# Attention and two feed-forward blocks on one core: another order of the work, a later copy of the pooled part, and shifted tiles for the last product

## What is computed

```python
out_d = sm_attn(mean4(q), mean4(k), mean4(v))        # attention on 144 pooled positions
attn  = repeat(out_d, 4) + sm_attn(q, k, v, |i - j| < 4)   # plus a local band
u     = x + real(fft(fft(x, axis=1), axis=2))         # x: attn as (4, 576, 512)
y     = u + relu(layernorm(u) @ w_ch1) @ w_ch2        # 512 -> 2048 -> 512
h     = relu(y @ w_in)                                # 512 -> 1024
out   = (h * sigmoid(conv3(h, conv_w))) @ w_out       # 1024 -> 512
```

## Time and profile before

| | us |
|---|---|
| median of 3 runs | 821.42 |
| the three runs | 818.27, 821.73, 821.42 |
| the profiled execution | 818.24 |
| its span, first to last instruction | 816.4 |
| PE busy | 804.5 |
| DVE busy | 447.4 |
| ACT busy | 299.3 |
| POOL busy | 269.8 |

### The profile page before, as it was taken

One profiled execution on the slowest core, in us unless ns is written; L12 is line 12 of the kernel. 1 busy time (PEld: TensorE's weight loads), 2 busy tenths in 40 slices (PEclk: granted clock), 3 DMA queues, 4 the chain that ended last, 5 costly groups with the idle time before them and its releaser, 6 DMA issues.

```text
span 816.4 us, 15990 instructions
## 1 busy us (share of the span) xinstructions
PE 804.5 (99%) x6414; PEld 730.0 (89%) x6414; DVE 447.4 (55%) x862; ACT 299.3 (37%) x879; POOL 269.8 (33%) x363
## 2 busy tenths in 40 slices
...
GB/s 187 230 138 136 45 107 56 70 62 86 61 16 107 38 102 4 155 26 1 28 54 214 62 1 64 1 65 0 65 1 1 1 53 1 64 2 1 53 1 65
DMA packets 79666, 49.52 MB, mean 61 GB/s; under 512 B 60240, under 2 KB 69480, under 8 KB 79592
## 3 DMA queue, kind: packets, MB, share of 16 engines
...
## 4 chain that ended last, share of the span: by engine, by line
PE 96%; DVE 2%; ACT 1%; issue 0%; POOL 0%; DVEq 0%; ACTq 0%
PE banks L834 14%; PE banks L851 14%; PE banks L969 12%; PE banks L986 12%; PE banks L928 11%; PE banks L943 11%; PE banks L792 4%; PE banks L734 3%; PE banks L662 2%; PE banks L648 2%; PE banks L695 2%; PE banks L761 1%; PE banks L681 1%; PE banks L719 1%; PE banks L707 1%; PE banks L821 1%
## 5 line engine op out<-in xcount | busy, mean ns | idle before, releaser
L1524 DVE SCALAR_TENSOR_TENSOR hw<-banks,hw 128x512 fp32r<-128x512 f32 x32 | 22.1, 692 | 122.1 <-ACT hw L1151 122.1
L834 PE MATMUL banks<-unH,w1aH 128*128 128x256 f32 x288 | 86.1, 299 | 0.6 <-DVE hL L1385 0.6
L851 PE MATMUL banks<-hH,w2aH 128*128 128x256 f32 x288 | 86.7, 301 | 0.0
L834 PE MATMUL banks<-unL,w1aH 128*128 128x256 f32 x288 | 81.3, 282 | 0.0
L834 PE MATMUL banks<-unH,w1aL 128*128 128x256 f32 x288 | 81.3, 282 | 0.0
L851 PE MATMUL banks<-hL,w2aH 128*128 128x256 f32 x288 | 81.3, 282 | 0.0
L851 PE MATMUL banks<-hH,w2aL 128*128 128x256 f32 x288 | 81.3, 282 | 0.0
L928 PE MATMUL banks<-unw,w1bH 128*128 128x512 f32 x256 | 78.9, 389 | 0.0
L943 PE MATMUL banks<-hw,w2bH 128*128 128x512 f32 x256 | 78.8, 389 | 0.0
L1754 POOL TENSOR_TENSOR accw<-accw,rstd_bc 128x512 f32<-128x512 f32 (+1 forms) x20 | 23.6, 1205 | 166.0 <-DVE remL L1581 85.2
L1385 DVE SCALAR_TENSOR_TENSOR hL<-banks,hH 128x256 fp32r<-128x256 f32 x80 | 33.7, 422 | 79.8 <-ACT hH L1082 79.7
...
## 6 DMA issues: line engine op xcount, KB each, us to landing
...
```

Source lines behind the costliest of these rows:

```text
L834: last = nc.tensor.matmul(bank[0][:, 0:CT], w[wp][:, t, P * m:P * m + P], (unH, unL)[xp][:, t, :], start=(t == 0 and i == 0), stop=(t == P ...
L851: last = nc.tensor.matmul(bank[1 + d // 2][:, CT * (d % 2):CT * (d % 2) + CT], w[wp][:, m, P * d:P * d + P], (hH, hL)[xp][:, m % 2, :], st ...
```

## The change

Four edits:

- PLAN is another order of the same stages. It has 39 filler matmuls where there were 44; all other stages are there once, as before. The first lines of both orders and the stretch around fold.3 are shown.
- For pairs 4 to 15 weigh.n.0 no longer waits for up_kept, and keep_up waits for weigh.n.0's end (pv_ready) in turn. X is then read by ACT only after both products are written.
- UW = 4 says from which pair on.
- hgH and all behind it move up in SBUF until hgH lies at the weights' place within 512 bytes.

```diff
@@ -85,132 +85,132 @@
-    load_q.0 load_k.0 load_c.0 load_c.1 warm.9 flip_q.0 keep_q.0 load_q.1 pool_q.0 warm.3 flip_k.0 keep_k.0 load_k.1
-    pool_k.0 warm.3 score.0.0 load_vg.0 load_vw.0 score.0.1 mask.0.0 top_l.0.0 score_d.0 mask.0.1 exp_l.0.0 flip_q.1
-    top_l.0.1 load_w1.0.0 load_q.2 keep_q.1 invert.0.0 top_d.0 norm_l.0.0 exp_l.0.1 warm.4 flip_k.1 keep_k.1 pool_v.0
...
-    top_l.4.0 score.4.1 keep_p1.3 fold.2 keep_p0.3 exp_l.4.0 score_d.4 mask.4.1 flip_pd.3 top_l.4.1 top_d.4 keep_pd.3
-    centre_w1.0.2 exp_d.4 warm.3 flip_q.5 load_q.6 invert.4.0 keep_q.5 warm.1 pooled.3 centre_w1.0.3 load_w2.0.0
-    flip_k.5 keep_up.3 exp_l.4.1 norm_l.4.0 weigh.3.0 pool_q.5 pool_v.4 keep_k.5 join.3.0 warm.3 flip_p.4.0 invert.4.1
-    weigh.3.1 pool_k.5 norm_l.4.1 score.5.0 load_vw.5 join.3.1 fold.3 norm_d.4 score_d.5 round_w2.0.0 flip_p.4.1
-    score.5.1 load_w2.0.1 keep_p1.4 top_d.5 load_k.6 keep_p0.4 fold_d.0.0 exp_d.5 load_vg.5 fold_d.0.1 load_w2.0.2
-    warm.4 flip_pd.4 keep_pd.4 mask.5.0 warm.3 pooled.4 top_l.5.0 mask.5.1 flip_q.6 keep_up.4 fold_q.0.0 weigh.4.0
-    keep_q.6 load_q.7 fold_s.0 feat.0.0.0 exp_l.5.0 top_l.5.1 feat.0.1.0 fold_d.0.2 round_w2.0.1 feat.0.2.0
-    keep_cos.0.0 fold_q.0.1 flip_k.6 exp_l.5.1 pool_v.5 keep_cos.0.1 load_k.7 feat.0.0.1 keep_cos.0.2 pool_q.6
...
+    load_q.0 load_k.0 load_c.0 warm.9 flip_q.0 keep_q.0 load_q.1 pool_q.0 warm.3 flip_k.0 keep_k.0 load_k.1 pool_k.0
+    warm.3 score.0.0 load_vg.0 load_vw.0 score.0.1 mask.0.0 top_l.0.0 score_d.0 mask.0.1 exp_l.0.0 flip_q.1 top_l.0.1
+    top_d.0 keep_q.1 invert.0.0 exp_l.0.1 norm_l.0.0 warm.4 flip_k.1 pool_q.1 load_k.2 keep_k.1 pool_v.0 pool_k.1
...
+    centre_w1.0.2 norm_l.4.0 pooled.3 keep_q.5 load_q.6 fold_d.0.0 keep_up.3 flip_k.5 pool_q.5 exp_l.4.1 weigh.3.0
+    load_k.6 keep_k.5 join.3.0 load_c.2 warm.1 flip_p.4.0 pool_k.5 weigh.3.1 invert.4.1 score.5.0 join.3.1 load_vw.5
+    norm_l.4.1 keep_p0.4 score_d.5 norm_d.4 centre_w1.0.3 flip_p.4.1 pool_v.4 score.5.1 keep_p1.4 mask.5.0 flip_pd.4
+    top_d.5 keep_pd.4 mask.5.1 top_l.5.0 load_vg.5 exp_d.5 warm.3 flip_q.6 fold.3 keep_q.6 warm.1 pooled.4 exp_l.5.0
+    weigh.4.0 fold_d.0.1 flip_k.6 fold_q.0.0 round_w1.0.1 fold_s.0 warm.2 feat.0.0.0 keep_up.4 keep_k.6 feat.0.1.0
+    keep_cos.0.0 score.6.0 fold_d.0.2 score.6.1 invert.5.0 fold_q.0.1 feat.0.2.0 norm_l.5.0 top_l.5.1 feat.0.0.1
...
+    relu.1.7 low_u.2.2 exp_l.10.1 keep_k.11 load_vw.10 pooled.9 invert.10.0 weigh.9.0 split.1.7 pool_v.11 score.11.0
+    keep_up.9 join.9.0 score.11.1 low_u.2.3 weigh.9.1 mask.11.0 norm_l.10.0 expand.2.0 invert.10.1 load_vg.12
...
@@ -239,6 +239,8 @@
     DR = LT + DG
 
     PQ = 8
+
+    UW = 4
     PB = D // P
     NP = B * PB
     HS = S // 2
@@ -397,6 +399,8 @@
         REM = S - FULL * P
         SF = FULL * P
         NG = 4
+
+        top[0] += (wa_at - top[0]) % 512
         hgH = sb("hgH", [P, NG, SF], F32R)
         hgL = sb("hgL", [P, NG, SF], F32R)
         remH = sb("remH", [P, M2, 2 * REM], F32R)
@@ -724,7 +728,8 @@
 
                 pe.wait_ge(vw_loaded[n % 2], 16 * 4 * (n // 2 + 1))
                 if g == 0:
-                    pe.wait_ge(up_kept, n + 1)
+                    if n < UW:
+                        pe.wait_ge(up_kept, n + 1)
                     pe.wait_ge(p_kept_v, n + 1)
                 else:
                     pe.wait_ge(x_done, 2 * n + 1)
@@ -1040,6 +1045,8 @@
 
             def keep_up(n):
                 act.wait_ge(up_ready, n + 1)
+                if n >= UW:
+                    act.wait_ge(pv_ready, 2 * n + 1)
                 at_least(act, x_done, 2 * n)
                 nc.scalar.mul(up[:], X[:, UP:UP + Sd], 1.0 / FACTOR).then_inc(up_kept, 1)
 
```

More of the change, by code:

```diff
@@ L92 @@
[L92 to L101, removed]
@@ L112 @@
[L112 to L121, removed]
@@ L122 @@
[L122 to L131, removed]
@@ L147 @@
-    score_d.11 invert.10.1 relu.2.0 load_k.12 keep_p0.10 norm_l.10.1 contract.1.7 top_l.11.0 norm_d.10 split.2.0
-    top_d.11 fold.9 flip_p.10.1 keep_acc.1 expand.2.1 keep_p1.10 exp_d.11 top_l.11.1 flip_pd.10 relu.2.1 contract.2.0
-    keep_pd.10 split.2.1 exp_l.11.0 pooled.10 flip_q.12 expand.2.2 keep_q.12 load_q.13 keep_up.10 pool_q.12 load_vg.11
-    flip_k.12 relu.2.2 exp_l.11.1 weigh.10.0 keep_k.12 load_k.13 contract.2.1 invert.11.0 store_acc.1 join.10.0
-    norm_l.11.0 invert.11.1 weigh.10.1 pool_k.12 norm_l.11.1 score.12.0 join.10.1 norm_d.11 score.12.1 mask.12.0
@@ L152 @@
-    split.2.2 score_d.12 pool_v.11 mask.12.1 flip_p.11.0 top_l.12.0 top_d.12 flip_p.11.1 expand.2.3 keep_p1.11
-    keep_p0.11 fold.10 exp_d.12 load_vg.12 flip_pd.11 contract.2.2 keep_pd.11 relu.2.3 split.2.3 pooled.11 expand.2.4
-    keep_up.11 weigh.11.0 relu.2.4 fold_d.2.0 contract.2.3 split.2.4 join.11.0 top_l.12.1 weigh.11.1 expand.2.5
-    join.11.1 fold.11 flip_q.13 relu.2.5 contract.2.4 keep_q.13 load_q.14 split.2.5 load_vw.12 flip_k.13 fold_d.2.1
-    expand.2.6 fold_q.2.0 keep_k.13 feat.2.0.0 relu.2.6 exp_l.12.0 fold_s.2 feat.2.1.0 split.2.6 fold_d.2.2
@@ new lines @@
+    norm_l.0.1 flip_p.0.0 top_d.1 load_vw.1 norm_d.0 flip_p.0.1 keep_p0.0 keep_p1.0 mask.1.1 warm.2 flip_pd.0
+    top_l.1.1 load_w1.0.0 invert.1.0 load_w1.0.1 keep_pd.0 norm_l.1.0 exp_d.1 warm.3 pooled.0 flip_q.2 pool_v.1
+    keep_up.0 keep_q.2 load_q.3 weigh.0.0 exp_l.1.1 flip_k.2 join.0.0 weigh.0.1 keep_k.2 load_k.3 score.2.0 load_vg.2
+    invert.1.1 load_w2.0.0 flip_p.1.0 join.0.1 norm_l.1.1 mask.2.0 keep_p0.1 norm_d.1 warm.1 flip_p.1.1 score.2.1
+    top_l.2.0 keep_p1.1 fold.0 pool_q.2 exp_l.2.0 flip_pd.1 pool_k.2 flip_cw mask.2.1 score_d.2 keep_pd.1 keep_cw
@@ new lines @@
+    top_l.2.1 flip_q.3 invert.2.0 top_d.2 pooled.1 keep_q.3 keep_up.1 flip_k.3 pool_q.3 exp_d.2 weigh.1.0 load_k.4
+    keep_k.3 norm_l.2.0 exp_l.2.1 join.1.0 score.3.0 load_q.4 pool_v.2 pool_k.3 score.3.1 mask.3.0 score_d.3 top_l.3.0
+    round_w2.0.0 invert.2.1 weigh.1.1 top_d.3 norm_l.2.1 exp_l.3.0 load_vg.3 flip_p.2.0 mask.3.1 load_vw.2 norm_d.2
+    flip_p.2.1 join.1.1 wmeans.0.0 keep_p0.2 keep_p1.2 fold.1 exp_d.3 top_l.3.1 invert.3.0 load_w1.0.2 low_w2.0.0
+    load_w2.0.1 exp_l.3.1 load_w1.0.3 flip_pd.2 centre_w1.0.0 keep_pd.2 invert.3.1 warm.3 pooled.2 centre_w1.0.1
@@ new lines @@
+    split.0.0 load_k.9 keep_k.8 expand.0.1 load_vg.7 exp_l.7.0 pool_k.8 load_vw.7 low_w1.0.1 contract.0.0 relu.0.1
+    split.0.1 pooled.6 load_q.9 invert.7.0 top_l.7.1 weigh.6.0 expand.0.2 keep_up.6 join.6.0 pool_q.8 low_w1.0.2
+    weigh.6.1 relu.0.2 exp_l.7.1 score.8.0 join.6.1 norm_l.7.0 score.8.1 mask.8.0 score_d.8 mask.8.1 round_w2.0.2
+    invert.7.1 contract.0.1 split.0.2 norm_l.7.1 round_w1.0.3 norm_d.7 flip_p.7.0 expand.0.3 pool_v.7 keep_p0.7
+    top_d.8 flip_p.7.1 contract.0.2 keep_p1.7 fold.6 relu.0.3 exp_d.8 split.0.3 flip_pd.7 low_w2.0.2 expand.0.4
```

175 lines of the change are left out of this document (100 added, 75 removed).

## The result

| | before | after |
|---|---|---|
| median, us | 821.14 (4 runs, 818.27 to 821.73) | 809.58 (4 runs, 809.40 to 809.73) |
| ratio of the times | | 0.9869 (95% interval 0.9845 to 0.9894) |
| profiled execution, us | 818.24 | 809.43 |
| its span | 816.4 | 807.6 |

The changed kernel is 1.3% faster, 11.6 us in the medians and 8.8 us between the two profiled executions. The forecast was 811.5, range 807 to 817, "faster" at 0.85; the sum behind it said 7.4 us between profiled executions.

A forecast was written before the change was run, and what follows sets the result against it. From about 110 us PE's own work was taken as the bound. Gains of 2.9 + 3.7 + 0.8 = 7.4 us off the profiled 818.24 gave 810.8; the median was put at 811.5, range 807 to 817.

The forecast's parts named there:

- two losses in front: Before feat.0.0.0: 44 filler matmuls with 15.3 us busy, and flip_pd.4's wait with slow clock and four fillers, 5.9 us together.
- Part 1: Last stage: aligning hgH and the tiles behind it cuts 6.6 ns from each of 432 matmuls, 2.9 us, bounds 0 to 2.9.
- Part 2: Front of the plan: fewer fillers, fold.3 behind keep_p0.4 and flip_k.6 ahead of feat gain 3.7 us, bounds 0.5 to 6.
- rival C: Near 62 us: late fold.3 leaves PE gaps, the clock falls to 0.53 again, feat no earlier; 815.2 us, chance 0.18.
- Part 3: Pairs 4 on: the changed wait on up, worth 0 itself, lets pooled and weigh stand together; 0.8 us, bounds -2 to 1.2.
- changeovers: On PE, a product behind another kind costs 0.08 or 0.09 us extra; fewer of these in the new list save 1.0 us.
- B: Last stage: the offset does nothing, the 6.6 ns coming from the weights being the moving operand; 814.4 us, chance 0.15.
- E: Last stage and front: B and C at once, so neither offset nor front gains; 818.1 us, chance 0.07.
- D: Twelve later pairs: keep_up late in ACT's queue makes PE wait 1.1 us each, 13 us; 824.7 us, chance 0.05.

## Why the prediction was right, and where its terms were off

**What bounds it.** Right: PE's own work, two losses in front, and the pitch of the last stage. The 8.8 us are 5.0 ahead of feat, 1.1 from there to the wide stage and 2.7 in the last stage.

**Part 1**, 2.9 us predicted, 2.7 measured (206.77 to 204.07). 432 matmuls by 0.2333 - 0.2268 = 6.5 ns is 2.8. The step that could have failed, that the place of the stationary tiles carries the 6.6 ns, held. The grid was stated wrongly (a multiple of 128) and turned out to be 256. The prediction set against this part the Trainium skill, "SBUF — State Buffer", section "Door 1: The DMA port swizzle", and worked out from its 16-byte lines that 288 bytes cost nothing. For this stage the measurement decides otherwise: 288, 64 and 32 bytes are all whole numbers of such lines, and each of them costs 6.5 ns.

**Part 2**, 3.7 predicted, 5.0 measured to feat.0.0.0, so the forecast's largest miss, 1.3 us:
- up to join.3.1's end 1.2 was predicted and 1.0 measured (57.64 to 56.65);
- from there to feat 9.5 us for 11.4, gain 1.9; measured 64.59 - 56.65 = 7.9, gain 3.4. The mis-sized term is fold.3: I took a middle between 4.9 and 2.6 us (the 9.5 leave about 4 for it), and it took 2.3. Its row had a minimum of 0.45 us for one of its first operations and 1.85 at the most; the choice between them was open because I had read POOL beside it without asking what POOL would hold beside it in the new order. In after POOL works on pool_v beside it only until 61.45 and is idle from there to fold.3's end at 62.70. What stands ahead of fold.3 on DVE was right: 3.85 us predicted, 3.8 measured (56.65 to 60.41);
- flip_k.6 ahead of feat: 0.6, as predicted (63.56).
That makes 5.0 of the 4.4 us by which feat is earlier and the 0.6 of flip_k.6. The wait of 2.96 us is gone, the clock is 1.00, and no gap is over 0.43 us from 55 to 66 us, so rival C is out. Of the parts of this gain, the runs isolate only fold.3's move; the 1.0 us up to join.3.1's end, put down to four fillers fewer, was not tested by itself.

**Part 3**, 0.8 predicted, 1.1 measured. From feat to the wide stage it is 366.49 us before and 364.84 after, 1.65 less, of which 0.55 are flip_k.6's. The wait on up is worth nothing in the old order, as said: there it was hidden. But it is worth 6.5 us in the new one, where weigh stands straight behind pooled; so the edit doesn't save a wait but pays for an order that would otherwise have it twelve times. The 1.1 us are what is left after a new wait of 1.3 us on score_d.8, which the prediction only named as "some new order will wait somewhere". That the gain of this stretch is the changeovers is argued from the counts in the prediction. No run changes their number alone, and it stays unshown.

**From the profiled execution to the median.** The sum gave 810.8 and the profiled execution was 809.4. I had then added 0.7 because the median of before lay 3.2 over its profiled run, and took that spread to stay. This was the step that failed in kind, if little in size: the spread of before came mostly from the clock behind the wait that the change removes, and the median of after is 0.15 from its profiled execution.

**Rivals.** B (offset does nothing), C (front no shorter) and E are excluded by the pitch and by the timeline. D, slower through a late keep_up, does not show in after: PE is busy for 319.83 us of the 320 from 110 to 430 us. Its mechanism exists though. In the UW = 0 variant a keep_up that waits at the head of ACT's queue does hold PE up, twice and by 0.9 us more than in after each time, and with the clock 5.3 us are lost; it is the sparse front in which that decides, not the twelve later pairs.
